# Attention, routed experts and an MLP on one core: the transposed probabilities become the fixed operand of the value product

## The chip, the cores and the metric

The kernel runs on one core of a Trainium2 chip. The metric is the device time of one execution in microseconds (us). Three runs of the kernel before are given, with their median, and one further execution was taken under the profiler. All engines named here belong to the same core: TensorE (PE in the profile, with its weight loads as PEld), VectorE (DVE), ScalarE (ACT), GpSimd (POOL) and SyncE (SP, which only issues transfers here).

## The reference

Three stages follow each other; the second needs every row of the first, and the third every row of the second.

```
scores_l = scale * q @ k.T, kept where |i - j| < 16       # local window
scores_s = scale * q @ k_blockmax.T + log(32)             # 24 block summaries
a = softmax(concat(scores_l, scores_s))                   # / (sum + 1e-9)
attn = a @ concat(v, v_blockmean)                         # B=2, H=8, S=768, D=64
x = attn as (B*S, H*D) = (1536, 512)
e(t) = argmax of (x/|x|) @ (emb/|emb|).T ; gate = its softmax probability
y[t] = gate * relu(x[t] @ w1[e]) @ w2[e]                  # 8 experts, 512 -> 1024 -> 512
h = y @ w_in ; g = P(h) / (Q(|h|) + 1e-6) ; out = g @ w_out   # 512 -> 2048 -> 512
```

All is in float32. The large products run as three passes over "high" and "low" halves of type float32r.

## The kernel before

**Attention.** The 1536 query rows are taken in NT = 12 tiles T of 128 rows. A tile has four pairs of heads, so that the stage consists of 48 units u = 4T + p. A query row meets KEYS = 182 keys: 24 block summaries and a window of LOC = 158 local rows. On PE a unit goes through three steps, and three units are in flight at a time: `scores(u)`, then `transposes(u - 2)`, then `products(u - 3)`, with `query_stack` (four transposes of query rows) in every odd unit.

- `scores` (L1581) makes both heads' 182 scores per query in one bank, each head in two passes, over the keys (KW) and the keys with their halves swapped (KWs).
- `scored` on DVE (L1127) adds the mask and finds the maximum; `exponent` on ACT (L830) writes the exponentials to `es` and their sum.
- `transposes` (line 1512 of the helper) turns the exponentials into columns: for each head 128 keys and then the last 54 (padded to 128), four in all; `copy_pt` (L1135 on DVE, L837 on ACT, by turns) brings 512 columns to PT.
- `products` (L1606, L1607) takes the values as the fixed operand: VA holds the 24 means and the first 104 local rows for all heads, VB the last 54. PT moves, 256 columns a time, and the result is x transposed, of which half of each block is used (head i of a pair only on its own 64 partitions). A float32 product is two passes on PE.
- `out_half` (L843, L1141) copies that to OT; `rows_of_x` transposes OT back and `make_x` (L1160) divides by the sums, giving x by token; `logits` (L1624) multiplies OT by the embedding EB for each pair of heads, and `make_logits` (L1166, L1169) scales and adds up the eight heads. `best`, `chosen`, `ranks` and `place` find a token's expert and its slot; `scatter` on POOL (L662) writes the row of x to its slot in DRAM.

Each engine runs its own list in the order in which it is written; semaphores are all that couples them. So a wait holds everything behind it on its engine. POOL prepares the keys of a tile (`windows`, L602 for the block maxima and L604 for the local keys), splits the query rows (L576, L579), and splits the first expert's weights (`split_slab0`, L614, L616, in tiles 3 to 9) from what `load_raw` fetched. SP makes KWs by a transfer inside the core (`swap_windows`, L447, L448), and loads values (`load_v`), value means (`load_means`) and queries. The slots in DRAM are cleared before the first scatter by three transfers (`zero_part`, L454), and `scatter(0)` in POOL's tile 5 waits for all three; the windows of tile 5 stand behind it.

**Set-up.** PE transposes the keys, sums the values over blocks of 32 (`value_sums`, L1526), and transposes the block maxima of the keys (`key_maxima`). The maxima of the second third of the keys are what POOL's first `windows` wait for.

**The rest.** From some 180 us on the experts' tiles and the last MLP follow. This part is not touched.

## Time and profile before

| | us |
|---|---|
| median of 3 runs | 713.1 |
| lowest, highest | 707.41, 714.42 |
| the profiled execution | 710.13 |
| its span, first to last instruction | 708.6 |
| PE busy in it | 676.5 (95%) |
| DVE, ACT, POOL busy | 491.1, 409.8, 162.3 |

PE is busy nearly throughout. A busy PE in this profile is one with a matmul in flight, and a matmul's duration (285 ns for 128 columns) is longer than the time until the next one starts, since they are pipelined. What a matmul costs is thus read from start to start. The timeline merges neighbours: "x4" in a row stands for four instructions, and what they take is the difference to the next row's start. PE's clock is granted at one of two levels, 2.4 GHz (1.00) and 1.2 GHz (0.50).

### The profile page before, as it was taken

What the parts mean: (1) busy time and instruction counts of PE and PEld (TensorE: products, weight loads), DVE (VectorE), ACT (ScalarE), POOL (GpSimd) and SP (SyncE); (2) the same over time, 40 slices, a digit from 0 to 9 for tenths busy, and PEclk for the clock granted to TensorE, in tenths of its full rate; (3) what the DMA queues carried; (4) which work ended last, traced back from release to release, by engine and by line L of the source; (5) the groups of instructions that cost most, each with busy time, mean ns of one, the idle gap of its engine ahead of it and who ended that gap; (6) DMA issues with size and microseconds to landing.
All of it is one profiled execution on the core that took longest, in us unless ns stands there. A gap on an engine that the chain in (4) does not pass through costs nothing.

```text
span 708.6 us, 11258 instructions
## 1 busy us (share of the span) xinstructions
PE 676.5 (95%) x3326; PEld 539.2 (76%) x3326; DVE 491.1 (69%) x981; ACT 409.8 (58%) x774; POOL 162.3 (23%) x213
## 2 busy tenths in 40 slices
PE   5889889999779999999999999999999999999997
PEld 5567667777668778888888888888888888888885
DVE  6856636766747798313323447999989899898886
ACT  7545536564446677433434446876666666676664
POOL 3449599621411002230100300101011000020000
PEclk9979979999989999999999999999999999999999
DMA  8679879741975799328413610100001000010001
GB/s 298 151 191 275 218 196 221 167 110 50 320 282 211 275 361 376 103 47 275 172 46 97 223 68 31 45 1 30 16 16 59 1 16 0 1 60 1 1 0 59
DMA packets 57906, 89.80 MB, mean 127 GB/s; under 512 B 32352, under 2 KB 32368, under 8 KB 56696
## 3 DMA queue, kind: packets, MB, share of 16 engines
q1 hardware_dynamic: 49880, 64.91, 30.2%
q0 software_dynamic: 7520, 24.15, 10.5%
q8 instruction: 30, 0.49, 0.3%
q14 instruction: 28, 0.23, 0.1%
q10 hardware_dynamic: 448, 0.02, 0.1%
HBM read 63.50 MB, written 16.63 MB: 113 GB/s over the span
## 4 chain that ended last, share of the span: by engine, by line
PE 84%; DMA 6%; DVE 3%; ACT 2%; POOL 1%; issue 1%; SPq 1%; ACTq 0%; POOLq 0%; DVEq 0%
PE bank L1779 19%; PE bank L1794 18%; PE bank L1742 13%; PE bank L1721 13%; PE bank L1512 9%; PE bank L1607 4%; PE bank L1581 3%; PE bank L1606 3%; PE bank L1624 2%; DMA x_by_slot<-x_all 1%; DMA kraw<-in_k_dram 1%; DMA raw_late<-in_moe_w_dram 1%; DMA xg<-x_by_slot 1%; PE bank L1526 1%; DVE weights L1259 1%
## 5 line engine op out<-in xcount | busy, mean ns | idle before, releaser
L1779 PE MATMUL bank<-X2T,weights 128*128 128x512 f32 x576 | 143.1, 398 | 0.0
L1794 PE MATMUL bank<-weights,G 128*128 128x512 f32 x576 | 139.4, 391 | 1.8 <-DVE G L1259 1.8
L1794 PEld LDWEIGHTS bank<-weights,G 128*128 128x128 f32 x576 | 108.1, 188 | 26.3 <-DVE G L1259 2.6
L1779 PEld LDWEIGHTS bank<-X2T,weights 128*128 128x128 f32 x576 | 107.8, 188 | 24.8
L1742 PE MATMUL bank<-weights,HT 128*128 (+1 forms) x456 | 113.3, 404 | 1.1 <-DVE HT L1259 1.1
L1721 PE MATMUL bank<-weights,XT 128*128 (+1 forms) x432 | 108.7, 401 | 3.4 <-DVE weights L1259 2.7
L1742 PEld LDWEIGHTS bank<-weights,HT 128*128 128x128 f32 x456 | 85.9, 192 | 20.9 <-issue 1.3
L1721 PEld LDWEIGHTS bank<-weights,XT 128*128 128x128 f32 x432 | 79.7, 188 | 22.9 <-issue 4.3
L933 ACT ACTIVATE qd<-bank,coef 128x512 f32<-128x512 f32 x48 | 33.1, 689 | 75.9 <-PE bank L1779 75.7
L830 ACT ACTIVATE es<-es,nmx 128x182 f32<-128x182 f32 x96 | 42.5, 443 | 58.1 <-DVE nmx L1127 57.9
L1259 DVE TENSOR_TENSOR HT<-bank,HT 128x512 fp32r<-128x512 f32 x38 | 24.4, 685 | 62.4 <-ACT HT L961 62.4
L1127 DVE CUSTOM_DVE_ANT_0 es<-bank,mask 128x182 f32<-128x182 f32 x96 | 31.3, 339 | 36.8 <-PE bank L1581 36.4
L1259 DVE TENSOR_TENSOR weights<-raw_late,weights 128x2048 f32 (+2 forms) x20 | 41.3, 2076 | 19.3 <-ACT weights L881 19.3
L704 POOL DMA_DIRECT2D y_in_order<-yo x19 | 10.6, 559 | 188.3 <-ACT yo L989 173.0
L1403 DVE SCALAR_TENSOR_TENSOR qd<-sq,absb,qd 128x512 f32<-128x512 f32 x48 | 36.0, 751 | 23.1 <-ACT sq L934 23.0
L1259 DVE TENSOR_TENSOR weights<-raw_early,weights 128x2048 f32 (+2 forms) x20 | 40.8, 2076 | 10.4 <-ACT weights L881 7.5
L881 ACT CAST weights<-raw_late 128x2048 f32 (+1 forms) x16 | 30.4, 1914 | 17.2 <-DMA raw_late<-in_moe_w_dram 17.2
L941 ACT ACTIVATE pb<-bank,ncoef 128x512 f32<-128x512 f32 x48 | 37.8, 788 | 0.0
L961 ACT CAST HT<-bank 128x512 fp32r<-128x512 f32 x36 | 19.4, 591 | 31.2 <-PE bank L1512 31.2
L1420 DVE SCALAR_TENSOR_TENSOR pb<-pb,ncoef,rr 128x512 f32<-128x512 f32 x48 | 36.1, 752 | 1.7
L1413 DVE SCALAR_TENSOR_TENSOR pb<-pb,ncoef,bank 128x512 f32<-128x512 f32 x48 | 35.9, 748 | 1.7
L943 ACT ACTIVATE rr<-qd,onep 128x512 f32<-128x512 f32 x48 | 34.7, 724 | 1.5 <-DVE qd L1403 1.5
(244 smaller groups left out, 1136.7 us busy)
## 6 DMA issues: line engine op xcount, KB each, us to landing
raw_early<-in_moe_w_dram SPq DMA_DIRECT2D x14, 1024.0 KB, 6.4
raw_late<-in_moe_w_dram SPq DMA_DIRECT2D x14, 1024.0 KB, 8.7
KWs<-KW SPq DMA_DIRECT2D x48, 182.0 KB, 4.5
y_in_order<-yo POOLq DMA_DIRECT2D x19, 256.0 KB
xg<-x_by_slot POOLq DMA_DIRECT2D x18, 256.0 KB, 6.1
x_all<-in_moe_w_dram POOLq DMA_DIRECT2D x8, 512.0 KB, 6.4
qraw<-in_q_dram SPq DMA_DIRECT2D x12, 256.0 KB, 5.1
VA<-in_v_dram SPq DMA_DIRECT2D x10, 208.0 KB
```

Source lines behind the costliest of these rows:

```text
L830: A_.activation(e_, e_, ACT.Exp, bias=nmx[:, slot:slot + 1], scale=-1.0, accum_out=sums[:, T % 2, 2 * p + i:2 * p + i + 1]).then_inc(exp_d ...
L941: A_.activation(pb[s], h, ACT.Identity, bias=ncoef[:, 2:3], scale=ncoef[:, 3:4]).then_inc(lin_done, 1)
L943: A_.activation(rr[:, s, :], qd[:, s, :], ACT.Ln, bias=onep[:, 0:1]).then_inc(ln_done, 1)
L1259: return V.tensor_tensor(out_, src, hi.bitcast(F32), ALU.subtract)
L1403: V.scalar_tensor_tensor(q_, h2, absb[:, 1:2], q_, ALU.mult, ALU.add).then_inc(q_done, 1)
L1413: V.scalar_tensor_tensor(g_, g_, ncoef[:, 1:2], h, ALU.add, ALU.mult).then_inc(h_read, 1)
L1420: V.scalar_tensor_tensor(g_, g_, ncoef[:, 0:1], r_, ALU.add, ALU.mult).then_inc(g_sb, 1)
L1512: return T_.transpose(dst, src, ident[0:rows, 0:rows])
L1721: last = T_.matmul(bank[half][:, :], x_t(i)[:, xa, kc * P:(kc + 1) * P], weights(par, wa, kc * F + half * BANK), start=(kc == 0 and n_ == ...
L1742: last = T_.matmul(bank[5][:, :], HT[:, ha, fc * P:(fc + 1) * P], weights(par, wa, KC * F + fc * DM), start=(fc == 0 and n_ == 0), stop=(f ...
L1779: last = T_.matmul(bank[6 + f % 2][:, :], W[:, 0, wa, kc * F2 + f * P:kc * F2 + (f + 1) * P], X2T[c % 2][:, xa, kc * C_TOK:(kc + 1) * C_TO ...
L1794: last = T_.matmul(bank[tt][:, :], G[:, f % 2, ga, tt * P:(tt + 1) * P], W[:, 1, wa, f * DM:(f + 1) * DM], start=(f == 0 and n_ == 0), sto ...
```

## The change

- In `products` the transposed probabilities are the fixed operand, and the values move: for each head 64 columns of VA, and then one product of 128 columns for both heads' last 54 keys (108 partitions). The result is x by token, in one bank of its own for each tile (4 or 5 by turns).
- So that one product can serve both heads, the second head of a pair has its keys in another order: in KW, `es` and the mask the first head has the summaries first and the last 54 local keys at its end, the second head its first 54 local keys first and the summaries last. `transposes` has three instead of four, `copy_pt` 384 instead of 512 columns. VB is cleared first and is block-diagonal in effect: each head's rows have values in its own columns only. `load_v` and `load_means` issue one transfer for each parity of head.
- `out_half`, `rows_of_x`, OT, EB and the scaling of the logits go. `make_x` reads the products' bank; `x_columns` transposes x on PE and ACT copies it to xT; `logits` takes xT, and its result needs no scaling.
- `windows` copies the block maxima only in the first two tiles of a batch.
- Order in the set-up: the second `value_sums` is cut in two around `key_maxima(1)`; `load_means` stands ahead of `swap_windows(1, ...)`; the three `zero_part` stand earlier; `mean_v(2)` stands ahead of `load_raw`; `place_embedding` ahead of `key_max(0)`.

```diff
@@ products, transposes, x_columns, logits (PE)
-                for part in range(2):
-                    for i in range(2):
-                        s = 2 * part + i
-                        last = transpose(bank[2 + u % 2][:, s * P:(s + 1) * P],
-                                         es[:, u % 3, i * KEYS + part * P:i * KEYS + (part + 1) * P])
+                transpose(bank[2 + u % 2][:, 0:P], es[:, u % 3, 0:P])
+                transpose(bank[2 + u % 2][:, P:2 * P], es[:, u % 3, P + 2 * KB:2 * KEYS])
+                last = transpose(bank[2 + u % 2][0:2 * KB, 2 * P:3 * P], es[:, u % 3, P:P + 2 * KB])
...
-                T_.matmul(O_, VA[:, r, p * P:(p + 1) * P], PT[:, u % 2, 0:2 * P], start=True, stop=False)
-                T_.matmul(O_, VB[0:KB, r, p * P:(p + 1) * P], PT[0:KB, u % 2, 2 * P:4 * P], start=False, stop=True)\
-                  .then_inc(pv_mm, 1)
+                    if T >= 2:
+                        pe.wait_ge(x_done, T - 1)
+                O_ = bank[4 + r]
+                for i in range(2):
+                    h = 2 * p + i
+                    T_.matmul(O_[:, h * D:(h + 1) * D], PT[:, u % 2, i * P:(i + 1) * P], VA[:, r, h * D:(h + 1) * D],
+                              start=(i == 0), stop=False)
+                T_.matmul(O_[:, p * P:(p + 1) * P], PT[0:2 * KB, u % 2, 2 * P:3 * P], VB[0:2 * KB, r, p * P:(p + 1) * P],
+                          start=False, stop=True).then_inc(pv_mm, 1)
...
+                pe.wait_ge(x_done, T + 1)
+                for kc in range(KC):
+                    last = transpose(bank[x_bank(T)][:, kc * P:(kc + 1) * P], x_all[:, T, kc * P:(kc + 1) * P])
...
+                pe.wait_ge(xt_done, T + 1)
+                for kc in range(KC):
+                    last = T_.matmul(bank[7][:, 0:E], xT[:, T % 2, kc, :], ET[:, kc, :],
+                                     start=(kc == 0), stop=(kc == KC - 1))
@@ ACT
-                if u % 4 in (0, 2) and 4 <= u < UNITS + 4:
-                    out_half(u // 4 - 1, u % 4 // 2)
+                if u % 4 == 0 and 8 <= u:
+                    x_columns(u // 4 - 2)
@@ DVE
+                if u % 4 == 3 and u >= 7:
+                    make_x(u // 4 - 1)
...
-                if u % 4 in (0, 2) and 4 <= u < UNITS + 4:
-                    out_half(u // 4 - 1, u % 4 // 2)
@@ SP
             store_means(0)
             store_means(1)
+            load_means(0)
+            load_means(1)
             swap_windows(1, 0)
             swap_windows(1, 1)
-            load_means(0)
-            load_means(1)
             load_q(3)
             load_v_all(2)
+            zero_part(0)
...
+                if 0 < T - 1 < ZERO_PARTS:
+                    zero_part(T - 1)
                 load_v(T)
-                if T < 2 + ZERO_PARTS:
-                    zero_part(T - 2)
@@ PE, set-up
-            value_sums(0)
-            value_sums(1)
+            value_sums(0, 0, 4)
+            value_sums(1, 0, 2)
             key_maxima(1)
+            value_sums(1, 2, 4)
@@ POOL
+                if T % TB < 2:
+                    maxima = KSs[:, bh * NSUM:(bh + 4) * NSUM].rearrange("c (p i n) -> c p i n", p=2, i=2)
...
+            mean_v(2)
             load_raw(0)
             load_raw(1)
-            mean_v(2)
```

**PE before:** from the end of a tile's last unit, where `rows_of_x` transposes OT back, through the next even unit to the logits; `es` are the exponentials, PT their transposes.

```order
L1512 MATMUL bank<-ident,OT 128x128 x4
L1581 MATMUL bank<-KW,QS 128x182
L1581 MATMUL bank<-KWs,QS 128x182
L1581 MATMUL bank<-KW,QS 128x182
L1581 MATMUL bank<-KWs,QS 128x182
L1512 MATMUL bank<-ident,es 128x128 x4
L1606 MATMUL bank<-PT,VA 128x256
L1607 MATMUL bank<-PT,VB 128x256
L1640 MATMUL bank<-oh,upper 128x8
L1641 MATMUL bank<-seen,ones 128x8
L1624 MATMUL bank<-EB,OT 128x16 x4
```

Each unit has four transposes and two long products, and nothing in it waits for DVE or ACT to finish work of the unit just before.

**The same place on PE now,** with the transposes of x ahead of it and the semaphores that each row waits for.

```order
L1505 MATMUL bank<-ident,x_all 128x128 [waits x_done,xt_done,qs_act]
L1505 MATMUL bank<-ident,x_all 128x128 x3
L1575 MATMUL bank<-KW,QS 128x182 [waits kws_in00,s_read,kw_done,qs_act]
...
L1505 MATMUL bank<-ident,es 128x128 [waits pt_dve,exp_done]
L1505 MATMUL bank<-ident,es 128x128
L1505 MATMUL bank<-ident,es 108x128
L1600 MATMUL bank<-VA,PT 128x64 [waits pt_act]
L1600 MATMUL bank<-VA,PT 128x64
L1602 MATMUL bank<-VB,PT 128x128
L1639 MATMUL bank<-oh,upper 128x8 [waits seen_ready,slot_ready,oh_ready,qs_dve]
L1640 MATMUL bank<-seen,ones 128x8
L1623 MATMUL bank<-ET,xT 128x8 [waits xt_done,lg_read,qs_dve]
```

Two long products became three short ones, a transpose is gone, and two rows wait for other engines' work on the same tile: the transposes of x for `x_done` (DVE), the logits for `xt_done` (ACT).

**DVE now, the last unit of a tile,** where `make_x` writes x_all and so releases the transposes of x:

```order
L1134 ISA es,nmx<-bank,mask 128x182
L1134 ISA nmx 128x1
L1169 TENSOR_REDUCE top_97<-LG 128x1
L1170 SCALAR_TENSOR_TENSOR pick<-LG,top_97,bank 128x8
L1172 TENSOR_REDUCE first<-pick 128x1
L1134 ISA es,nmx<-bank,mask 128x182
L1134 ISA nmx 128x1
L1159 TENSOR_TENSOR x_all<-bank,rsum 128x512
L1128 CAST QS<-bank 128x512
```

Before, the copy to QS stood ahead of `make_x`, and nothing on PE waited for `make_x` within a unit.

**SP in the set-up, now** (KWs are the swapped keys of tiles 1 and 2, v_block_means the stored means, x_by_slot the slots to be cleared):

```order
L447 DMA v_block_means<-vmean 128x64 [waits vmean_ready] x2
L442 DMA VA<-v_block_means 24x4x64 [waits vm_out1,vm_out0]
L442 DMA VA<-v_block_means 24x4x64
...
L452 DMA KWs<-KW 64x728 [waits kw_done]
L453 DMA KWs<-KW 64x728
...
L412 DMA qraw<-in_q_dram 128x8x64 [waits q_split]
L406 DMA vraw_75<-in_v_dram 128x2048 [waits vm_mm]
L459 DMA x_by_slot<-x_all 128x4x512 [waits cleared]
```

The means, in four transfers instead of two, now stand ahead of the swapped keys of tile 1, and the first clearing stands right behind the load of the last third of the values, where before it stood eight rows later, behind the values of tile 2.

## Rows read from the trace of the kernel before

**Rows 1.** The page: the span.
```profile
span 708.6 us, 11258 instructions
```

**Rows 2.** Stretches: us; busy (x count) of PE, PEld, DVE, ACT, POOL; PE's clock; DMA.
```profile
106.20:148.90 42.70, 42.70 (x284) 32.11 (x281) 29.55 (x132) 26.23 (x92) 30.98 (x39) 1.00 0.75 177
```

**Rows 3.** Timeline of PE, two stretches: start us, us, engine, line, operation, count.
```profile
113.89 0.35 PE L1581 MATMUL bank<-KW,QS 128*128 128x182 f32 x1
...
116.85 0.33 PE L1581 MATMUL bank<-KW,QS 128*128 128x182 f32 x1
...
117.36 0.60 PE L1512 MATMUL bank<-ident,es 128*128 128x128 f32 x4
117.80 0.60 PE L1606 MATMUL bank<-PT,VA 128*128 128x256 f32 x2
118.33 0.70 PE L1607 MATMUL bank<-PT,VB 54*128 54x256 f32 x2
118.95 0.18 PE L1640 MATMUL bank<-oh,upper 128*128 128x8 bf16 x1
...
119.02 1.04 PE L1624 MATMUL bank<-EB,OT 128*128 128x16 f32 x8
119.91 0.33 PE L1581 MATMUL bank<-KW,QS 128*128 128x182 f32 x1
```

**Rows 4.** Timeline of DVE in the last unit of a tile, to the tile's make_x.
```profile
114.72 0.35 DVE L1127 CUSTOM_DVE_ANT_0 es<-bank,mask 128x182 f32<-128x182 f32 x1 [0.30 <-PE bank L1581]
...
115.64 0.35 DVE L1127 CUSTOM_DVE_ANT_0 es<-bank,mask 128x182 f32<-128x182 f32 x1
...
115.91 0.68 DVE L1121 CAST QS<-bank 128x512 fp32r<-128x512 f32 x1
117.19 0.69 DVE L1160 TENSOR_TENSOR x_all<-bank,rsum 128x512 f32<-128x512 f32 x1 [0.60 <-issue]
```

**Rows 5.** Timeline of ACT in the same unit.
```profile
115.11 0.45 ACT L830 ACTIVATE es<-es,nmx 128x182 f32<-128x182 f32 x1 [0.75 <-DVE nmx L1127]
...
115.56 0.56 ACT L837 COPY PT<-bank 128x512 f32<-128x512 f32 x1
```

**Rows 6.** Timeline of POOL: the scatters of tiles 0 and 1.
```profile
85.66 1.06 POOL L662 DMA_INDIRECT x_by_slot<-x_all,slot_id  x1 [7.41 <-DMA x_by_slot<-x_all]
...
95.19 1.04 POOL L662 DMA_INDIRECT x_by_slot<-x_all,slot_id  x1 [0.30 <-issue]
```

**Rows 7.** Timeline of PE: the first scores of tiles 4, 5 and 6.
```profile
75.55 0.33 PE L1581 MATMUL bank<-KW,QS 128*128 128x182 f32 x1
...
91.40 0.49 PE L1581 MATMUL bank<-KW,QS 128*128 128x182 f32 x1 [4.94 <-DMA KWs<-KW]
...
106.19 0.33 PE L1581 MATMUL bank<-KW,QS 128*128 128x182 f32 x1
```

**Rows 8.** Stretches, columns as in the second group: after the two falls of the clock.
```profile
38.40:49.00 10.60, 10.56 (x32) 6.95 (x32) 4.65 (x19) 3.96 (x14) 4.18 (x13) 0.52 0.79 194
...
91.40:100.20 8.80, 8.80 (x36) 7.38 (x36) 3.36 (x18) 2.08 (x8) 8.04 (x10) 0.50 0.88 225
```

**Rows 9.** Timeline of PE in the set-up: the second value sums.
```profile
22.85 3.60 PE L1526 MATMUL bank<-x_all,ident 128*128 128x512 f32 x8
```

**Rows 10.** The chain of waits in the set-up: start us, us, what; the means' way into VA.
```profile
35.01 3.30 DMA VA<-v_block_means
```

**Rows 11.** The page: DMA issues of the swapped keys, KB each, us to landing.
```profile
KWs<-KW SPq DMA_DIRECT2D x48, 182.0 KB, 4.5
```

**Rows 12.** Stretches, columns as in the second group: full clock, PE in pauses or at transposes.
```profile
31.80:35.20 3.40, 2.58 (x22) 2.37 (x22) 3.15 (x12) 2.30 (x9) 3.32 (x6) 1.00 0.69 179
36.40:38.40 2.00, 0.17 (x2) 0.00 (x0) 1.97 (x6) 0.74 (x3) 0.29 (x1) 1.00 0.98 227
...
13.80:17.60 3.80, 3.80 (x37) 3.72 (x36) 3.73 (x4) 3.80 (x9) 2.83 (x2) 1.00 1.01 418
174.90:178.70 3.80, 3.27 (x32) 3.02 (x32) 2.99 (x13) 0.44 (x2) 0.98 (x1) 1.00 0.83 239
```

More of the change, by code:

```diff
@@ L315, in heads, with pair_heads, x_bank @@
             return ap.rearrange("p (h d) -> p h d", h=H)
+        def pair_heads(ap, i):
+            return ap.rearrange("p (h i d) -> p h i d", h=PAIRS, i=2)[:, :, i, :]
+        def x_bank(T):
+            return 6 if T < NT - 1 else 2
         def expert_chunk(e, c):
@@ L420, in load_v, with rows @@
                 start = t * P - HALO
-                cut, mid, end = max(0, -start), start + LA, min(S, start + LOC)
-                split = mid if cut == 0 else FIRST_ROWS
-                at = NSUM + split - start
-                sp.dma_start(heads(VA[NSUM + cut:at, r, :]),
-                             v[b, :, start + cut:split, :].rearrange("h p d -> p h d")).then_inc(v_in[r], 16)
-                if split < mid:
-                    sp.dma_start(heads(VA[at:P, r, :]),
-                                 v[b, :, split:mid, :].rearrange("h p d -> p h d")).then_inc(v_in[r], 16)
-                sp.dma_start(heads(VB[0:end - mid, r, :]),
-                             v[b, :, mid:end, :].rearrange("h p d -> p h d")).then_inc(v_in[r], 16)
+                cut, end = max(0, -start), min(S, start + LOC)
+                def rows(to, at, parity, first, last):
+                    sp.dma_start(pair_heads(to[at:at + last - first, r, :], parity),
+                                 v[b].rearrange("(h i) s d -> i s h d", i=2)[parity, first:last]).then_inc(v_in[r], 16)
+                if cut > 0:
+                    rows(VA, NSUM + cut, 0, 0, FIRST_ROWS)
+                    rows(VA, NSUM + cut + FIRST_ROWS, 0, FIRST_ROWS, start + LA)
+                else:
+                    rows(VA, NSUM, 0, start, start + LA)
+                rows(VA, 0, 1, start + KB, end)
+                rows(VB, 0, 0, start + LA, end)
+                rows(VB, KB + cut, 1, start + cut, start + KB)
             def load_means(T):
@@ L1248, in _ @@
                     key_max(2, ROW // 8)
-                if u % 4 == 3 and u >= 7 and u < LOOPS - 1:
-                    make_x(u // 4 - 1)
             place(NT - 2)
@@ L1255, in _ @@
             chosen(NT - 1, bank[0])
-            make_x(NT - 1)
             place(NT - 1)
@@ L1521, in embedding, with value_sums @@
                 last.then_inc(eT_mm, 1)
-            def value_sums(g):
+            def value_sums(g, first, last):
                 pe.wait_ge(v_all_in[g], 16)
-                for j in range(4):
-                    last = T_.matmul(bank[(7, KT_BANKS)[g]][:, :], ident[:, :], vraw[g][:, j * BANK:(j + 1) * BANK],
+                for j in range(first, last):
+                    sum_ = T_.matmul(bank[(7, KT_BANKS)[g]][:, :], ident[:, :], vraw[g][:, j * BANK:(j + 1) * BANK],
                                      start=(j == 0), stop=(j == 3))
-                last.then_inc(vm_mm, 1)
+                if last == 4:
+                    sum_.then_inc(vm_mm, 1)
             def key_columns(g):
@@ L1559, in query_stack @@
                 if j == 0 and T >= 3:
-                    pe.wait_ge(x_done, T - 2)
+                    pe.wait_ge(xt_done, T - 2)
                 if v == 5:
@@ L1622, in logits @@
                     pe.wait_ge(lg_read, T)
-                for p in range(PAIRS):
-                    last = T_.matmul(bank[7][:, p * 2 * E:(p + 1) * 2 * E], OT[:, T % 2, p, :], EB[:, p, :],
-                                     start=True, stop=True)
+                pe.wait_ge(xt_done, T + 1)
+                for kc in range(KC):
+                    last = T_.matmul(bank[7][:, 0:E], xT[:, T % 2, kc, :], ET[:, kc, :],
+                                     start=(kc == 0), stop=(kc == KC - 1))
                 last.then_inc(lg_mm, 1)
@@ L1664, in _ @@
                     key_maxima(2)
-                if (u % 4 == 1 and 9 <= u < UNITS) or u == UNITS:
-                    T = (u - 9) // 4 if u < UNITS else NT - 2
+                if u % 4 == 1 and 9 <= u < UNITS:
+                    T = (u - 9) // 4
                     if T >= 1:
@@ L1700, in stored_rows @@
                               start=False, stop=False)
+            pe.wait_ge(slot_ready, NT - 1)
+            logits(NT - 1)
             first_rows(NT - 2)
```

110 lines of the change are left out of this document (46 added, 64 removed).

## The prediction

> **What bounds the kernel now.** I read the stretches first, then PE's timeline, then the chain of waits. In the attention stage PE has a matmul in flight in all of a stretch of 42.7 us that holds exactly four tiles [rows 2], while DVE, ACT and POOL are busy for 29.6, 26.2 and 31.0 us of it. So a tile costs 10.67 us, and PE's own work sets it. One unit shows what that work is, read from start to start [rows 3]: four score passes 0.51 us, four transposes of `es` 0.44, the VA product 0.53, the VB product 0.62. Eight logit passes with only 16 moving columns take 0.89, 0.11 each, no less than a transpose with 128 columns (0.44 / 4). So 0.11 us is the floor of one weight load with its matmul, and only the 256 columns of the products are above it. The VA product has two passes of 256 columns in 0.53 us and the VB product, which has 54 partitions, takes 0.09 more: there is a pause at the change of 128 to 54 partitions and back.
>
> The stage is not steady throughout. Tiles 4 and 5 take 106.19 - 75.55 = 30.6 us [rows 7], 9.3 more than two tiles of 10.67. The reason stands on POOL: `scatter(0)` waited 7.41 us for the clearing of the slots [rows 6], the windows of tile 5 stood behind it, and PE stood idle for 4.94 us until their swap landed [rows 7]; then its clock was at 0.50 for some 10 us [rows 8]. The set-up shows the same on a smaller scale: PE waited for the means until 38.4 us and then ran at half clock until 49.
>
> **The change, step by step.**
>
> *Products and transposes (PE).* Now three float32 products of two passes, 64, 64 and 128 columns. None is above the floor, so I take 6 x 0.11 = 0.66 us instead of 0.53 + 0.62 = 1.15, and 3 x 0.11 for the transposes instead of 0.44. A unit saves 0.49 + 0.11 = 0.60 us, a tile 2.4: 10.67 becomes 8.25 if nothing else waits. Unknown is whether 108 partitions pause as 54 do. The lower bound is 0, as with 128. The upper bound is all that the present two products take above their columns: eight passes of 512 columns have 3.60 us [rows 9], so 256 take 0.22, four such passes 0.9 and the pauses 1.15 - 0.9 = some 0.3 us a unit. I take 0, since the rows with 128 partitions around them stand without a pause and 108 is nearer to those than to 54; the range keeps the 0.3.
>
> The Trainium skill (TensorEngine Tiling (Array Packing), Key Properties) says that "Changing tiling mode (not just tile) drains the TensorE", with modes of 64 and 128 rows. By that rule 108 rows stay in the 128-row mode and the pause goes; without it the sum would keep the 0.3.
>
> *x by token (PE, DVE, ACT).* The transposes of x (4) and the logits (8 passes of 0.11) cost PE what they did. What is new are two waits per tile, because the work per unit is now shorter than the chains between engines.
>
> First wait, `x_done`. In the tile's last unit DVE starts `scored` 0.83 us after PE's first score pass (113.89 to 114.72, [rows 3, 4]); `best` and the second `scored` follow, and what comes next can start 1.19 later (115.91); that is now `make_x`, 0.69 us [rows 4]. x is there 0.83 + 1.19 + 0.69 = 2.71 us after the scores began. PE meanwhile has scores 0.51, queries 0.44, transposes 0.33, products 0.66 = 1.94. It stands 0.8 us.
>
> Second wait, `xt_done`. In the next unit ACT begins its first exponent 0.39 after `scored` (115.11 - 114.72), each exponent holds it for 0.45 (115.56 - 115.11), and then the copy to xT follows, which is as large as the present copy of PT, 0.56 [rows 5]: 0.83 + 0.39 + 0.45 + 0.45 + 0.56 = 2.68 us after the scores began. PE has 0.51 + 0.33 + 0.66 + 0.07 (ranks, 118.95 to 119.02) = 1.57. It stands 1.1 us.
>
> Together 1.9 us: the tile costs 8.25 + 1.9 = 10.15, and of the 2.4 us only 0.52 are left. Tiles 2 to 10, nine of them, give 9 x 0.52 = **4.7 us**. In the last tile three units' savings (1.8) stand against the new chain make_x, transposes, copy (0.69 + 0.44 + 0.56, handovers of 0.15) ahead of the last logits: 0.
>
> DVE and ACT lose the copies to OT and a quarter of the copies to PT. That is worth nothing by itself; it is slack on engines that were 69% and 61% busy in that stretch, and the two chains above are counted with it.
>
> *POOL.* Between scatters it takes 9.5 us a tile [rows 6], which is less than 10.15 and shrinks by two small copies. It does not bound, but it is only 0.6 us behind: were PE's waits gone, POOL would be the next bound in tiles 5 to 8.
>
> *Clearing earlier (SP).* The three clearings leave before the values of tiles 2 and 3 instead of after those of 2, 3 and 4, so the last lands well before POOL arrives at `scatter(0)`. POOL's work ahead of it ends at about 78.3 (85.66 - 7.41). The swapped keys of tile 5 then land at 91.4 - 7.4 = 84.0, or some 0.5 sooner with the maxima's copies gone. PE, with set-up and two tiles faster, wants them at about 71.7 + 10.2 = 81.9. So it still waits, some 1.7 us instead of 4.94, and I take the clock as staying up. What goes is the 9.3 us, what comes 1.7. Against that the first clearing (1 MB) now runs beside the load of the last third of the values, which `mean_v(2)` and the raw weights of POOL wait for: between 0 and 4 us on POOL's chain, I take 1. **9.3 - 1.7 - 1 = 6.6 us.**
>
> *Set-up.* `key_maxima(1)` moves ahead of half of the second value sums, 3.60 / 2 = 1.7 us [rows 9], and so do POOL's first windows and SP's first swap. The means landed 3.30 us after their issue at 35.01 [rows 10]; the issue now hangs on the store ahead and comes some 1.2 us sooner. Five units fall in the time until tile 2: 5 x 0.60 = 3.0. But the swap of tile 1 is queued behind four transfers of means: its keys land about 4.5 us after issue [rows 11], near 39.3, so PE waits 1.4 us behind its first products. 1.2 + 3.0 - 1.4 = **2.8 us**, between 0 and 4.3. The clock falls there again, since PE's pause of about 2 us stays.
>
> *Sum.* 4.7 + 6.6 + 2.8 = 14.1 us. All of it shifts the experts' stage, whose first rows wait for the last scatter; that stage is unchanged. The profiled execution took 710.1 us (its span is 708.6 [rows 1]) and gives 696.0. It lies 3.0 under the median of the runs, and between the lowest and the median, so I put the forecast between 696.0 and 713.1 - 14.1 = 699.0: **697.5 us**.
>
> **The rivals.**
>
> *A, the waits hardly come* (8%). DVE and ACT have more slack than before and might be earlier than in the rows. Then POOL bounds tiles 5 to 8 at about 9.1 and PE the other five at 8.25: 4 x 1.05 + 5 x 1.9 = 13.7 more, 684. Against it: both chains are read without any queue ahead of them, so they are already the shortest.
>
> *B, 108 partitions pause too* (12%). 0.3 a unit, but in two of a tile's four units it is hidden in the waits: 0.6 x 9 = 5.4, with the set-up 6: 703.
>
> *C, slower: the clock falls within the steady tiles* (10%). The two waits stand 2.1 us apart, so PE idles 1.9 us in about 4, and what it does is short. For it: the clock fell after 36.4 to 38.4, where PE was busy 0.17 of 2.00 us [rows 12]. Against it: it stayed at 1.00 where PE was busy 2.58 of 3.40, with nothing but transposes (3.80 of 3.80), and at the short logit and rank passes of 174.9 to 178.7 (3.27 of 3.80) [rows 12]. A tile at half clock is 2 x 8.25 = 16.5 us, and the waits vanish in it: 6.3 more than 10.15. The 14.1 are gone after 2.2 such tiles, slower by over 1% from 3.4 on; with seven it is 697.5 + 44 = 742.
>
> The Trainium skill (TensorE: Matmul & The Clock Gate, Part 4) says that transposes do not count as PE-busy in the same way and that the full clock does not engage for them. By that rule this change, which leaves mostly transposes and short products, would go to C's 742; the full clock through 3.8 us of transposes alone speaks against it.
>
> *D, the clock falls once more before tile 5, or POOL's chain is later by the full 4 us* (17%). 5 us for one fall (10 us at half, [rows 8]), 3 for the chain: 701 to 706.
>
> The forecast itself has 53%, 692 to 701.
>
> **How the numbers follow.** About 1% (7 us) can be told from no change: faster is below 706.0, slower above 720.2. The forecast, A, B and most of D are faster, with something left off for what I have not seen: 0.80. The rest of D, and C with two to four tiles, is within 1%: 0.12. C beyond that: 0.08. The range reaches down into part of A and up to D's end: 687 to 707.
>
> **What would show it.** Right: products in six passes 0.11 apart; PE idle about 0.8 us ahead of the transposes of x and about 1.1 ahead of the logits in each tile; tiles of 10.1 to 10.3 us; no wait of POOL for the clearing; tile 6 beginning near 95 instead of 106.2 us. Wrong: tiles near 8.3 or 9.1 (A), starts of the VB product later than 0.11 (B), a clock under 0.9 anywhere between 50 and 165 us (C, D).

## The result, and the profile after

Over 20 runs each the kernel before took a median of 709.1 us (699.4 to 719.4) and the changed kernel 703.1 us (697.5 to 710.9). The ratio is 0.993, with a 95% interval of 0.990 to 0.996; all ratios here are taken over the fast runs alone (within 1.5% of the kernel's fastest), so that they differ a little from those of the medians. The gain is 6 us where the forecast had 14. The profiled execution took 698.8 us; its page has:

```profile
span 697.2 us, 11272 instructions
...
KWs<-KW SPq DMA_DIRECT2D x48, 182.0 KB, 3.5
```

The span is to be compared with [rows 1]; the swapped keys land 3.5 us after their issue by the median, 4.5 in [rows 11]. The next rows are stretches (us; busy time and count of PE, PEld, DVE, ACT, POOL; PE's clock; DMA): four steady tiles, then the half clock in tile 2, and tile 1 with the wait behind it.

```profile
106.70:147.70 41.00, 33.49 (x300) 32.54 (x298) 23.76 (x121) 24.65 (x88) 23.42 (x25) 1.00 0.62 164
51.60:61.80 10.20, 9.94 (x47) 9.67 (x48) 2.69 (x17) 4.12 (x14) 9.35 (x12) 0.50 0.91 244
37.84:51.52 13.68, 9.76 (x66) 8.94 (x66) 7.88 (x28) 5.27 (x20) 8.10 (x16) 0.88 1.02 307
```

A steady tile costs 41.00 / 4 = 10.25 us instead of 10.67 [rows 2], and PE is no longer busy all the time: 33.49 of 41.00. Its timeline shows the logits of the tile before, then a plain unit, and the end of the tile up to the next one's first scores:

```profile
138.97 0.17 PE L1640 MATMUL bank<-seen,ones 128*128 128x8 bf16 x1
140.28 1.03 PE L1623 MATMUL bank<-ET,xT 128*128 128x8 f32 x8 [1.14 <-ACT xT L852]
...
143.02 0.33 PE L1575 MATMUL bank<-KW,QS 128*128 128x182 f32 x1
...
143.52 0.49 PE L1505 MATMUL bank<-ident,es 128*128 128x128 f32 x3
143.85 0.56 PE L1600 MATMUL bank<-VA,PT 128*128 128x64 f32 x4
144.25 0.44 PE L1602 MATMUL bank<-VB,PT 108*128 108x128 f32 x2
144.44 0.33 PE L1575 MATMUL bank<-KW,QS 128*128 128x182 f32 x1
...
146.11 0.44 PE L1602 MATMUL bank<-VB,PT 108*128 108x128 f32 x2
147.28 0.63 PE L1505 MATMUL bank<-ident,x_all 128*128 128x128 f32 x4 [0.73 <-DVE x_all L1159]
147.66 0.33 PE L1575 MATMUL bank<-KW,QS 128*128 128x182 f32 x1
```

From the first transpose's start to the next scores is 144.44 - 143.52 = 0.92 us for three transposes and six product passes, where the unit of before had 1.59 (117.36 to 118.95, [rows 3]). The products take 144.44 - 143.85 = 0.59 us, a tenth each. The two waits stand where the forecast put them: 0.73 us ahead of the transposes of x, 1.14 ahead of the logits. POOL's timeline at the place of [rows 6]:

```profile
75.62 1.06 POOL L671 DMA_INDIRECT x_by_slot<-x_all,slot_id  x1 [0.31 <-issue]
...
84.77 1.03 POOL L671 DMA_INDIRECT x_by_slot<-x_all,slot_id  x1 [0.30 <-issue]
```

`scatter(0)` no longer waits for the clearing, and is issued 10 us earlier. What is new is ahead of tile 2. PE's timeline, SP's queue and the chain of waits there:

```profile
47.59 0.60 PE L1505 MATMUL bank<-ident,x_all 128*128 128x128 f32 x4
51.52 0.38 PE L1575 MATMUL bank<-KW,QS 128*128 128x182 f32 x1 [3.32 <-DMA KWs<-KW]
```

```profile
37.18 0.67 SPq L406 DMA_DIRECT2D vraw<-in_v_dram  x1
37.90 0.45 SPq L459 DMA_DIRECT2D x_by_slot<-x_all  x1
...
38.95 1.00 SPq L453 DMA_DIRECT2D KWs<-KW  x1
...
44.15 3.92 SPq L459 DMA_DIRECT2D x_by_slot<-x_all  x1
48.11 3.97 SPq L423 DMA_DIRECT2D VA<-in_v_dram  x2
```

```profile
38.95 12.32 DMA KWs<-KW
```

The keys of tile 2 (182 KB) land 12.3 us after their issue, behind 1 MB of values and 1 MB of clearing; PE stands 3.32 us for them and then has half clock for ten, as the row 51.60:61.80 above shows. SP itself is held for 3.9 us at the second clearing and as long at the values of tile 2.

**Where the time went.** Two profiles of each kernel (that of [rows 1] with r1's below, the one above with r2's), cut at the first scores of tiles 2, 4, 6 and 11 and at the start of the last scatter, give for before and after, in us:

| piece | before | changed | mean difference | forecast |
|---|---|---|---|---|
| start to tile 2 | 54.3, 49.6 | 51.5, 51.7 | -0.3 | -2.8 |
| tiles 2 and 3 | 21.3, 21.3 | 24.2, 24.3 | +3.0 | 0 |
| tiles 4 and 5 | 30.6, 34.2 | 20.4, 22.8 | -10.8 | -8.6 |
| tiles 6 to 10 | 53.3, 53.3 | 51.5, 51.4 | -1.9 | -2.6 |
| tile 11 to the last scatter | 19.9, 20.4 | 20.3, 20.6 | +0.3 | 0 |
| the rest, to the end of the span | 529.2, 529.4 | 529.2, 531.3 | +0.9 | 0 |

The last column cuts the prediction's sum at the same places (set-up -2.8; collision +1 and two tiles at -0.5; clearing -9.3 + 1.7 and two tiles; five tiles). Nearly all of the miss, 5.5 us, lies before tile 4. Of it the 3.0 us in tiles 2 and 3 repeat in both pairs of profiles; the 2.5 us before tile 2 are less sure, since there the two profiles of the kernel before differ by 4.7 us.

### The profile page after: what moved, and what is told of

Same layout as the page of the kernel before. It is cut to its first block, busy times and chain, and to the rows that moved or that the text cites. A ratio compares the mean times of both kernels' runs of the same rounds, so it can differ in the third digit from the quotient of the medians.

```text
span 697.2 us, 11272 instructions
## 1 busy us (share of the span) xinstructions
PE 648.4 (93%) x3374; PEld 542.1 (78%) x3374; DVE 475.6 (68%) x944; ACT 405.2 (58%) x762; POOL 158.1 (23%) x205
## 3 DMA queue, kind: packets, MB, share of 16 engines
q0 software_dynamic: 7520, 24.15, 10.5%
## 4 chain that ended last, share of the span: by engine, by line
PE 77%; DMA 8%; DVE 6%; ACT 5%; issue 3%; SPq 1%; DVEq 0%; POOL 0%; ACTq 0%; POOLq 0%
PE bank L1780 19%; PE bank L1795 18%; PE bank L1743 12%; PE bank L1722 12%; PE bank L1505 6%; PE bank L1575 3%; DMA raw_late<-in_moe_w_dram 3%; DMA KWs<-KW 2%; PE bank L1623 2%; ACT weights L891 2%; DVE weights L1252 2%; ACT es L839 1%; PE bank L1600 1%; DMA raw_early<-in_moe_w_dram 1%; DMA kraw<-in_k_dram 1%
## 5 line engine op out<-in xcount | busy, mean ns | idle before, releaser
L1743 PE MATMUL bank<-weights,HT 128*128 (+1 forms) x456 | 111.2, 398 | 1.4 <-DVE HT L1252 1.4
L1743 PEld LDWEIGHTS bank<-weights,HT 128*128 128x128 f32 x456 | 84.2, 188 | 20.9 <-issue 1.8
L943 ACT ACTIVATE qd<-bank,coef 128x512 f32<-128x512 f32 x48 | 33.1, 689 | 75.7 <-PE bank L1780 75.6
L1134 DVE CUSTOM_DVE_ANT_0 es<-bank,mask 128x182 f32<-128x182 f32 x96 | 31.4, 339 | 51.5 <-PE bank L1575 49.7
```

What stands on the lines that cost most here:

```text
L1743: last = T_.matmul(bank[5][:, :], HT[:, ha, fc * P:(fc + 1) * P], weights(par, wa, KC * F + fc * DM), start=(fc == 0 and n_ == 0), stop=(f ...
```

## The experiments

After the two traces my theory was: the clearing ahead of tile 2's keys makes them late, the pause brings the half clock, and the two waits keep what the products save. The rival: the tiles before the fourth are bound by transfers and POOL anyway, whatever the order and the clock.

Times are medians; each ratio is to the kernel before in the same job, with its 95% interval. Of each run one execution was profiled, so that a place in time rests on one profile, and two profiles of one kernel can differ by some us there.

**Both kernels again** (no edit).

> The kernel before, unchanged, for a second profile. If the forecast missed because single executions scatter by where the clock falls, this one shows tiles of 10.67 us again but its pauses and its stretches at half clock at other places or of other length than the first. If the first profile was typical, 708 to 711 us with the same two falls.

> The changed kernel, unchanged. The first profile (span 697.2) lay at the low end of its 20 runs (697.5 to 710.9, median 703.1). Theory 1 (the pause at tile 2, behind the earlier clearing, and the clock that falls with it, differ from run to run): tiles stay at 10.23 us, median near 703, and the half-clock time of this profile differs from 30 us. Theory 2 (the steady tiles vary): tiles other than 10.23 us.

r1: 710.8 us, 1.001 (0.997 to 1.004). r2: 702.6 us, 0.988 (0.984 to 0.992). In r1's profile the steady tiles cost the same 10.68 us, but the half clock lies elsewhere: there is none between 38 and 49 us, and the one from tile 5 on lasts from 86.6 to 103.6 us instead of 90 to 100. So the falls of the clock vary from run to run of the kernel before, and the forecast was worked out from one profile of it. The changed kernel's second profile repeats the steady tiles (51.4 us for five), the late tile 4 (76.0) and the pause ahead of tile 2:

```profile
51.66 0.32 PE L1575 MATMUL bank<-KW,QS 128*128 128x182 f32 x1 [2.64 <-DMA KWs<-KW]
```

So the late tile 4 is not one run's accident. This profile has one fall more than the first, half clock from 81 to 88 us in tile 4. Between jobs the gain of the change is 6 to 8 us.

**The two parts alone.** r3 is the change with the set-up order of before, r4 the kernel before with the new set-up order; r15 and r13 repeat them. The edit that r3 takes back and r4 makes alone (shown without `place_embedding` and without the definition of `value_sums`):

```diff
-            swap_windows(1, 0)
-            swap_windows(1, 1)
             load_means(0)
             load_means(1)
+            swap_windows(1, 0)
+            swap_windows(1, 1)
             load_q(3)
             load_v_all(2)
+            zero_part(0)
...
+                if 0 < T - 1 < ZERO_PARTS:
+                    zero_part(T - 1)
                 load_v(T)
-                if T < 2 + ZERO_PARTS:
-                    zero_part(T - 2)
...
+            mean_v(2)
             load_raw(0)
             load_raw(1)
-            mean_v(2)
...
-            value_sums(0)
-            value_sums(1)
+            value_sums(0, 0, 4)
+            value_sums(1, 0, 2)
             key_maxima(1)
+            value_sums(1, 2, 4)
```

> The changed kernel with the set-up order of before (swap of tile 1 before the means, clearing after the values of tiles 2, 3 and 4, mean_v(2) after load_raw, value sums in one piece). Theory 1 (the new order gives much: no wait of POOL for the clearing): slower than the change by 5 to 8 us, with POOL waiting 5 to 7 us ahead of scatter(0). Rival (the new order takes back at tile 2 what it gives at tile 5): within 2 us of the change.

> The kernel before with only the new set-up order. By theory 1 6 to 9 us faster than before (no pause before tile 5, full clock there); by the rival (a pause at tile 2 instead, behind the earlier clearing) 0 to 3 us faster.

> The kernel before with the new set-up order alone, once more. Theory (the set-up order gives its gain on the old attention, and the changed attention pays it back in half clock and pauses): 9 to 10 us below before again, tile 6 starts at 94 to 95 us, no half clock from 50 to 165 us. Rival (the first run was a lucky one for the clock): half clock shows in attention as in the profiles of the kernel before, tile 6 starts at 98 or later, and the time is 3 to 6 us below before.

> The changed attention with the set-up order of before, once more. Theory: 6 to 7 us below before again, half clock in tiles 1 to 5 and a pause at tile 4, tile 6 at 101 to 103 us. Rival (chance of the clock): a profile without half clock between 50 and 165 us, tile 6 at 98 or earlier, 9 us or more below before.

r4: 700.4 us, 0.988 (0.984 to 0.992). r13: 702.4 us, 0.988 (0.984 to 0.992). r3: 703.4 us, 0.991 (0.988 to 0.993). r15: 704.6 us, 0.992 (0.989 to 0.995). So the new order alone gives 8 to 10 us, the new attention alone 6 to 7, and both together, r2 in r3's and r4's job, 7.4; by the ratios both together (0.988) are worth what the order alone is. The parts do not add, and neither theory expected that: r3 came 0.8 us behind the change instead of 5 to 8, as its rival had it, and r4 gained 9.6 instead of the rival's 0 to 3. Stretches of r13 (to tile 2, to tile 6, to tile 11, to the last scatter), then of r15 at the same places, and the second one of r4:

```profile
31.60:50.60 19.00, 15.84 (x98) 11.45 (x98) 14.94 (x52) 10.60 (x40) 11.94 (x22) 0.99 0.89 250
50.60:97.90 47.30, 47.30 (x279) 35.68 (x279) 28.69 (x129) 26.41 (x92) 40.83 (x50) 0.90 0.98 238
97.90:151.20 53.30, 53.30 (x352) 40.08 (x351) 36.90 (x165) 32.75 (x115) 32.02 (x40) 1.00 0.67 166
151.20:171.00 19.80, 19.27 (x131) 14.18 (x129) 14.17 (x67) 8.72 (x29) 3.46 (x4) 1.00 0.27 94
```

```profile
31.60:47.90 16.30, 13.41 (x102) 12.79 (x102) 13.70 (x50) 9.84 (x38) 11.54 (x24) 0.90 0.91 226
47.90:98.70 50.80, 39.66 (x298) 38.16 (x295) 23.57 (x119) 25.10 (x88) 40.05 (x44) 0.87 0.91 244
98.70:150.10 51.40, 41.73 (x373) 40.53 (x371) 29.66 (x151) 30.79 (x110) 31.80 (x36) 1.00 0.63 172
150.10:170.80 20.70, 16.73 (x134) 16.04 (x133) 10.33 (x58) 9.01 (x30) 3.46 (x4) 0.88 0.31 108
```

```profile
49.20:94.40 45.20, 43.39 (x279) 32.17 (x279) 29.00 (x130) 26.45 (x92) 40.36 (x48) 1.00 1.02 254
```

With the order of before, the new attention reaches tile 2 at 47.9 and 49.3 (r15, r3) and tile 4 at 69.1 and 71.4; the old attention had 49.6 and 54.3, 70.9 and 75.6. By the means that is 3.4 us sooner at tile 2 and 3.0 at tile 4, near the 3.0 that the forecast gave the shorter units up to tile 2; but the profiles of each kernel differ by as much. With the new order both attentions come to tile 4 at 73 to 76.5 us (r4 72.8, r13 76.5, changed 75.8 and 76.0). The faster units are lost in it. From tile 6 on, r13's 53.30 + 19.80 = 73.1 against r15's 51.40 + 20.70 = 72.1 is all that the new attention is worth in the rest of the stage: 1 us. r15 still has the old pause, in the timelines of PE and POOL:

```profile
85.19 0.49 PE L1574 MATMUL bank<-KW,QS 128*128 128x182 f32 x1 [3.97 <-DMA KWs<-KW]
```

```profile
79.66 1.06 POOL L670 DMA_INDIRECT x_by_slot<-x_all,slot_id  x1 [6.85 <-PE bank L1504]
```

The releaser named there is a transpose of PE, long done; the wait is the one of [rows 6], for the clearing. As to the clock, r13 has the old attention and half clock from 50.2 to 60 (0.90 in its second row), where r4, the same kernel, had none (1.00 in all stretches, of which one is shown). So half clock does not come with the new attention alone. The pair also shows what one fall goes with: from tile 2 to tile 4 r4 took 72.8 - 49.2 = 23.6 us and r13 76.5 - 50.6 = 25.9. r13's theory had a gain of 9 to 10 us and no half clock, its rival 3 to 6 us with half clock; it gained 8.0 us with half clock, so that neither holds as a whole. r15 has half clock in tiles 1, 4 and 5 and is 5.8 us below before, near its theory's 6 to 7, but tile 6 begins at 98.7 us instead of 101 to 103.

**The two waits taken away (r5).** The transposes of x go behind the next unit's, the copy to xT ahead of the second exponent, the logits a unit later.

```diff
-                if u % 4 == 1 and 9 <= u < UNITS:
-                    T = (u - 9) // 4
+                if u % 4 == 2 and 10 <= u < UNITS:
+                    T = (u - 10) // 4
...
                     transposes(u - 2)
+                if u % 4 == 0 and 8 <= u:
+                    x_columns(u // 4 - 2)
...
-                if u % 4 == 3 and u >= 7:
-                    x_columns(u // 4 - 1)
```

> The change with the transposes of x moved behind the transposes of the next unit, the copy to xT ahead of the second exponent, and the logits one unit later, so that neither waits. Theory (the two waits of 0.7 and 1.1 us are what keeps a tile at 10.24 us): PE's waits ahead of x_all and logits gone, tiles of 8.3 to 9.2 us where POOL allows, 5 to 10 us faster than the change. Rival (another engine or POOL's windows bound as well): tiles stay above 9.5 us and 0 to 3 us are won.

r5: 694.1 us, 0.976 (0.970 to 0.980). Five tiles in the stretches, and in PE's timeline the transposes of x and the logits without a wait:

```profile
94.10:137.20 43.10, 41.90 (x371) 40.48 (x371) 28.27 (x148) 31.30 (x108) 31.92 (x36) 1.00 0.79 200
```

```profile
112.10 0.63 PE L1505 MATMUL bank<-ident,x_all 128*128 128x128 f32 x4
...
115.58 1.04 PE L1623 MATMUL bank<-ET,xT 128*128 128x8 f32 x8
```

A tile is 43.10 / 5 = 8.62 us, near the 8.25 that the prediction gave PE alone. Five tiles take 51.4 - 43.1 = 8.3 us less. The kernel's gain over r8 (below, the change but for its tail, 703.3 us in the same job) is 9.1. So these two waits are what held back the saving of the new products in the steady tiles, as r5's theory had it.

**The clearing later (r6), and with late x (r7).** Part 0 goes behind the values of tile 2, part 1 ahead of those of tile 3, part 2 behind them.

```diff
-            zero_part(0)
...
-                if 0 < T - 1 < ZERO_PARTS:
-                    zero_part(T - 1)
+                if T == 3:
+                    zero_part(1)
                 load_v(T)
+                if T in (2, 3):
+                    zero_part(2 * (T - 2))
```

> The change with only the clearing moved: behind the values of tile 2, ahead of and behind those of tile 3. Theory (the clearing issued ahead of tile 2's swapped keys makes them land 12 us after issue): they land within 8 us, PE's pause of 3.3 us before tile 2 is gone and tile 2 begins at 47 to 49 instead of 51.5 us; 3 to 5 us faster, if the last part still lands before scatter(0). Rival (the load of the values delays them, not the clearing): tile 2 still begins at 51 or later.

> Both edits. If they are independent, the sum of the two gains (8 to 14 us under the change). If POOL's windows bound, no more than the better of the two plus 2 us.

r6: 708.7 us, 0.996 (0.993 to 1.000); r7: 698.5 us, 0.982 (0.978 to 0.986). Both are slower than their partners of the same job, r8 and r5, by 5.4 and 4.4 us. Tile 2 paused only 1.2 us, but its keys were still late, now with the values' load alone ahead of them, and tile 4 paused 3.96. The chain of waits of r6:

```profile
38.53 0.69 SPq L406
...
39.80 10.34 DMA KWs<-KW
```

Without the clearing ahead, 10.3 of the 12.3 us are left. The clearing was not their main cause, and the theory, by which r6 was to gain 3 to 5 us, fell in this part. The values' load stands ahead of these keys in the order of before too, where they took 7.2 to 7.6 us in the profile of before and up to 10.5 in r3.

**Less to clear (r9), and with late x (r10).** Only the first 128 rows are cleared ahead, 0.25 MB instead of 3.25; the tail of expert 0 is cleared by the store that does this for the others. The clearing of the other rows is left out.

```diff
-        ZERO_PARTS = 3
+        ZERO_PARTS = 1
...
-                tiles = REGION // P
+                tiles = 1
...
-            for e in range(1, AHEAD + 1):
+            for e in range(0, AHEAD + 1):
                 clear_tail(e, zeroed)
```

> The change, with the clearing cut to what can be read: the first 128 rows of the first expert's slots (0.25 MB instead of 3.25 MB), and one more indirect store that clears the 128 rows behind its last one, as the other experts have. Theory (the 3.25 MB and the SP queue that they hold cost the change its lead at tiles 2 to 5): no pause over 1.5 us at tiles 2 to 5, tile 6 at 88 to 92 instead of 96 to 99 us, 4 to 7 us faster than the change in spite of the added store (1.3 us). Rival (what is in the way is the load of the values, which stays): tile 2 still pauses by 2 us or more and at most 2 us are won.

> The same with the later transposes of x and logits. If clearing and waits are independent causes: 12 to 15 us faster than the change, 687 to 691 us. If POOL's chain (9.1 us a tile) binds tiles 3 to 8 then, no more than 2 us over the kernel with the later transposes alone (694.1).

r9: 700.4 us, 0.991 (0.987 to 0.994), no better than the change. r10: 691.1 us, 0.978 (0.973 to 0.982), no better than r5 by its interval. (Its median lies at the edge of what independent causes were to give, 687 to 691, but in its job the kernel before was 4 us faster than in r5's.) In r9 the pause ahead of tile 2 fell to 0.80 us, yet tile 4 began at 77.2 and tile 6 at 97.7, where its theory had 88 to 92. The 3.25 MB cost little where they stand now.

**The keys first (r11), and all three together (r14).** Tile 2's keys go ahead of the values and of the clearing; r14 has r10's edits with it.

```diff
             load_q(3)
-            load_v_all(2)
-            zero_part(0)
             for T in range(2, NT):
                 swap_windows(T, 0)
                 swap_windows(T, 1)
+                if T == 2:
+                    load_v_all(2)
+                    zero_part(0)
```

> The change, with one difference on the queue: the load of the last third of the values and the clearing of part 0 are issued behind tile 2's swapped keys instead of ahead of them. Theory (what lies ahead in the queue makes these keys land 12 us after their issue): they land within 5 us, TensorE does not pause ahead of tile 2's first scores (3.3 us with the change), tile 2 starts at 46 to 48 us instead of 51.5; the mean of the values of tile 2 comes 3 to 4 us later, so tile 3 or 4 may pause instead and the total stays within 2 us of the change's. Rival (the keys are late for another reason, contention with the loads under way): they still take 9 us or more and tile 2 starts at 50 or later.

> The change with columns of x later and one product behind, only the first 128 rows cleared ahead (the clearing of the rest is left out, but for the last rows' store), and the last third of the values and that clearing behind tile 2's swapped keys. Theory (the pauses of tiles 2 and 3 move to the next thing that GpSimd makes late): within 2 us of 691 us, a pause of 2 to 4 us ahead of tile 3. Rival (they are separate losses and add): 687 us or less, tile 4 starts at 68 us or earlier, against 70.9 with the keys' order of the change.

r11: 702.6 us, 0.985 (0.980 to 0.990); r14: 690.3 us, 0.972 (0.969 to 0.976), which can't be told from r10's 0.978 (their intervals overlap from 0.973 to 0.976). In r11 tile 2's keys land 4.7 to 5.6 us after their issue and tile 2 starts without a pause at 47.9, 3.6 us sooner than in the change, and PE then stands as long ahead of tile 3:

```profile
47.86 0.33 PE L1576 MATMUL bank<-KW,QS 128*128 128x182 f32 x1
...
61.68 0.49 PE L1576 MATMUL bank<-KW,QS 128*128 128x182 f32 x1 [3.34 <-DMA KWs<-KW]
```

Which work makes tile 3's keys late is read from r14's chain (start us, us, what), which ends at the same scores, there after a pause of 5.29 us:

```profile
41.12 7.51 DMA vraw<-in_v_dram
...
48.70 2.38 POOL vraw L595
...
54.26 0.39 POOL vmean L598
...
56.08 0.73 POOL KW L615
...
57.34 4.88 DMA KWs<-KW
...
62.46 0.71 PE bank L1576 x2
```

It is one line: the last third of the values lands at 48.6, POOL's `mean_v(2)` takes until 54.7, two loads of raw weights are issued, the windows of tile 3 are cut, and their swap takes 4.9 us. So in this order tile 3 doesn't start before some 62 us, however early PE is. The other profiles bear it out: in r4, r5, r7, r9, r10, r11 and r14 PE stands 1.0 to 5.3 us ahead of tile 3, and the wait ends between 61.1 and 62.5 us in all seven. The rows of r4 and r14:

```profile
61.10 0.33 PE L1583 MATMUL bank<-KW,QS 128*128 128x182 f32 x1 [1.02 <-DMA KWs<-KW]
```

```profile
62.46 0.49 PE L1576 MATMUL bank<-KW,QS 128*128 128x182 f32 x1 [5.29 <-DMA KWs<-KW]
```

In r15, with `mean_v(2)` starting at 46.5 and the raw loads already issued ahead of it, tile 3 starts at 58.1. In the changed kernel itself nothing is seen of this bound: PE comes to tile 3 only at 65.5, after half clock until 61.8.

**PE kept busy in the pauses (r12), and in the tail (r8).** r12 adds transposes of the identity matrix ahead of the scores of tiles 1, 2 and 3, r8 seven matmuls with 512 columns behind tile 11; what they compute is not used.

```diff
+                if u in (4, 8, 12):
+                    for k in range({4: 10, 8: 24, 12: 10}[u]):
+                        transpose(bank[4 + u // 4 % 2][:, 0:P], ident[:, :])
```

```diff
+            def keep_busy(n):
+                pe.wait_ge(w0_ready, 2 * CHUNKS)
+                for k in range(n):
+                    T_.matmul(bank[3][:, :], W[:, 0, HI, 0:P], W[:, 0, HI, BANK:2 * BANK], start=True, stop=True)
...
+                if u == LOOPS - 1:
+                    keep_busy(4)
...
+            keep_busy(3)
```

> The change, with transposes of the identity matrix into an idle bank ahead of the first scores of tile 1 (10), tile 2 (24) and tile 3 (10), so that TensorE works where it paused; their results are not used. Theory (the half clock of 52 to 62 us follows from the pause ahead of tile 2, and costs some 5 us): the granted clock stays 1.00 from 38 to 76 us, tile 4 starts 2 to 5 us earlier than with the change, and the total is 2 to 5 us below it. Rival (tiles 3 and 4 wait for GpSimd's chain and for the swapped keys in any case): the clock stays up, but tile 5 starts where it did and the total is the change's within 1 us.

> The change with seven more matmuls of 512 columns into an unused bank, four ahead of the last tile's transposes of x and three ahead of its logits; their result is not used. Theory (the stretch behind the last unit is 3 us longer than before because PE's clock falls to half in its pauses): the clock stays at 1.00 until the experts' first product, and the stretch from the last unit's scores to it takes 13 to 14 us instead of 16.4; 2 to 3 us faster. Rival (the chain of x over DVE, PE and ACT is what is longer): still 15.5 to 17 us.

r12: 705.5 us, 0.988 (0.983 to 0.994); the same gain as the change within the intervals. PE's timeline in tile 2, and the stretch from its start to tile 3:

```profile
50.08 2.78 PE L1505 MATMUL bank<-ident 128*128 128x128 f32 x24
52.62 0.33 PE L1575 MATMUL bank<-KW,QS 128*128 128x182 f32 x1
...
55.47 1.08 PE L1623 MATMUL bank<-ET,xT 128*128 128x8 f32 x8 [1.18 <-ACT xT L852]
```

```profile
52.60:67.90 15.30, 14.12 (x85) 13.96 (x84) 5.62 (x28) 6.40 (x22) 13.57 (x17) 0.67 1.04 301
```

There is no pause ahead of tile 2, PE is busy 14.12 of 15.30 us behind it, and the clock is at 0.67 all the same (half from 56.3 to 66.5). The changed kernel's fall near 38 us is gone as well, but there is one from 46 to 49.5. Both falls are as long as there (3.4 and 10.2 us) and 5 to 8 us later. So the long pause ahead of tile 2 is not needed for the half clock, and the theory fell in this part too. The one wait left before the second fall is the usual one of 1.18 us ahead of the logits, which in the steady tiles comes with 1.00. r8: 703.3 us, 0.987 (0.983 to 0.991). Its tail had full clock and its first expert matmul came 15.5 us after the last unit's scores, against 18.2 in the changed kernel (15.1 and 16.2 in the two profiles of the kernel before), so that the theory holds for the tail; yet the 2 to 3 us that it was to be worth are not seen, the total being that of r2. From that matmul to the last one it took 526.1 us, against 521.2 in the changed kernel and 523.4 in r2. Why the stage behind gives the time back was not looked into.

## Why the prediction was wrong, step by step

- **Products and transposes**: right. 0.59 us for six passes against 0.66 taken and 1.15 before, and no pause with 108 partitions: the VB product stands 0.40 behind the VA product's four passes (143.85 to 144.25). Rival B is out. The Trainium skill's rule (TensorEngine Tiling (Array Packing), Key Properties) that a change of tiling mode drains TensorE would have it so; the traces agree, with no gap at 108 rows now and 0.09 us at 54 rows before.
- **The two waits**: right in place and size (0.8 and 1.1 forecast, 0.73 and 1.14 measured). Rival A is out for this kernel; r5 shows that a tile of 8.62 us was there to be had by moving x.
- **Steady tiles**: mechanism right, size a little high: 0.42 us a tile instead of 0.52. That it is so near is in part luck: the products saved 0.07 us a unit more than taken, and the waits, read from start to start as the products are, cost 0.97 (146.11 to 147.28, less 0.20 for two passes) and 1.28 us (138.97 to 140.28, less 0.03).
- **Clearing**: the wait of 7.41 us is gone, and tiles 4 and 5 gained 10.8 where 8.6 were forecast. The 1.7 us wait for tile 5's keys did not come, because tile 4 came 4 us later than the forecast had it (71.7); in r10, where it began at 70.9, PE stood 2.32 us ahead of tile 5. Tile 6 began at 96.2 and 98.8 us, where the forecast had some 95.
- **Set-up, to the start of tile 4**: this is the step that failed. "Five units fall in the time until tile 2", 3.0, with 1.2 for the means and -1.4 for tile 1's keys, was to give 2.8, and the load of the values beside the clearing was to cost 1. Tile 1's wait came as written (1.40 us), and with the set-up order of before the new attention was about 3 us ahead (r3, r15). But two things stood in no term of the sum. First, tile 2's keys: the forecast priced the queue for tile 1 and put tile 2's wait at nothing, and PE waited 3.32 us for them, 12.3 us after their issue. Most of that is the load of the values, which stands ahead of these keys in the old order too; the clearing adds some 2 us (r6). Second, the clock behind it: the sum has no fall after the one near 38 us, and tile 2, at half clock from 51.6 to 61.8, cost 14.0 us. Where these two were less, POOL's chain was the next bound: no sooner than 61.1 us was tile 3 let go after a wait in any profile of the new order, and the forecast had this chain as one microsecond of delay. The sum put PE's savings where PE was not the last to arrive: +2.7 instead of -2.8. Compared with the first profile alone tile 2 began just 2.8 us earlier (51.5 against 54.3), but that is chance: r1's began at 49.6.
- **The clock and rival D**: D (17%) said "the clock falls once more before tile 5, or POOL's chain is later by the full 4 us", 701 to 706. The first half of it came in both profiles of the change, with the sign given for it (half clock past 50 us), and the time, 703.1, lies in D's range. Rival C, that the clock falls within the steady tiles, is out as the cause of the miss, since tiles 6 to 10 have 1.00 in both profiles; but it can happen: r8 has a fall from 102 to 105.5 us and r12 one from 104 to 111. The fall forecast near 38 us came, for 3.4 us where before it was ten. What brings a fall is open: r4 and r13 are the same kernel with none and with one, and r12 had it without the long pause, so that the clock's share of the miss is not shown by a run that changes it alone. The Trainium skill (TensorE: Matmul & The Clock Gate, Part 4) has it that the full clock does not engage for transposes; the 3.80 us of nothing but transposes at 1.00 [rows 12] do not agree, and the steady tiles, which mix them with scores and short products, stay at 1.00 as well.
- **The tail**: forecast 0, measured +0.3 to the last scatter and +0.9 behind it, within the spread of the profiles. The chain used up the units' savings, as forecast: from the last unit's scores to the first expert matmul it is 18.2 us against 15.1 and 16.2, with half clock in the last part.

The sum by the rows of the table is 2.7 - 10.8 - 1.9 + 0.3 + 0.9 = -8.8 us for the profiles, and the gains of the runs' medians, 6 (the result) and 7.4 (r2's job), lie a little below. The best kernel of the study, r14, has 690.3 us, and r10 691.1: 2.8 and 2.2% below before in their jobs. What they have beyond the change comes from moving x, as r5 has it too.

## What to carry to other kernels

Before savings of one engine are counted per tile, ask of each tile which of its inputs arrives last: a steady-state saving is worth nothing in the tiles where a transfer or another engine's chain sets the start, here the first ones. Where an order of issue changes, follow every later item of that queue to who waits for it, not only the item next to the edit, and expect that mending one late input shows the next, as tile 3's keys in r11. Take a second profile of the kernel before ahead of the forecast: here it would have shown that the fall near 38 us and the start of tile 4 (75.6 or 70.9) are not fixed. When shorter work leaves an engine waiting on a round trip through two others, the cure is distance: issuing the dependent step one unit later was worth 9 us here, more than the change itself.

## What the runs showed of the hardware

A swapped-keys transfer of 182 KB took 4.7 to 5.6 us from issue to landing with no load of 1 MB just ahead of it in its queue (tile 2 in r11; 4.9 for tile 3 in r14), 7.2 to 7.6 behind one in the kernel before, 10.3 in r6 and 10.5 in r3, and 12.3 behind a load and a clearing of 1 MB each. Half clock appeared behind pauses of PE and also in r12 from 56.3 to 66.5 us, where PE was busy 92% of the tile and had stood 1.18 us shortly before; it was absent from one of two profiles of the same kernel (r4, r13). Two profiles of one kernel differ by up to 3.5 us in when tile 6 starts (94.4 in r4, 97.9 in r13).
